# SOLU's first product in plain float32 from the raw w_in, with a new order of the first stages

## What is computed

```python
def _moe2_ref(x, w_in, w_out, g_ln):          # x 1536 x 384, w_in 384 x 1024, w_out 1024 x 384
    h = x @ w_in
    h_max = np.max(h, axis=-1, keepdims=True)
    e = np.exp(h - h_max)
    sm = e / (np.sum(e, axis=-1, keepdims=True) + 1e-09)
    solu = h * sm
    mu = np.mean(solu, axis=-1, keepdims=True)
    var = np.mean((solu - mu) ** 2, axis=-1, keepdims=True)
    ln = (solu - mu) / np.sqrt(var + 1e-06) * g_ln
    return (ln @ w_out).astype(np.float32)
```

## Time and profile before

| | us |
|---|---|
| runs (3) | 338.69, 339.14, 339.18; median 339.14 |
| the profiled execution | 340.64 |
| its span, first to last instruction | 338.8 |
| PE busy in the span | 318.0 |
| DVE, ACT, POOL busy | 206.0, 197.3, 189.1 |
| mean granted TensorE clock | 0.992 of full |

### The profile page before, as it was taken

How to read it: one execution, slowest core, us unless ns; L and a number is a source line. 1 busy time by engine, 2 the same in 40 slices (tenths; PEclk the granted TensorE clock), 3 DMA queues, 4 the chain that set the end, 5 groups by cost and what they waited for, 6 DMA issues and landing times.

```text
span 338.8 us, 6574 instructions
## 1 busy us (share of the span) xinstructions
PE 318.0 (94%) x2390; PEld 281.5 (83%) x2390; DVE 206.0 (61%) x473; ACT 197.3 (58%) x377; POOL 189.1 (56%) x170
## 2 busy tenths in 40 slices
PE   5899999977899999999999999998999999999991
PEld 2688887853699999999999999786899999999991
DVE  4567667777545555464646556889966666666610
ACT  2578777675376758576666667455554555433520
POOL 6966597963895978879696959501111111111131
PEclk9999999999999999999999999999799999999998
DMA  9999999991994949393857593000000000000000
GB/s 128 164 281 267 250 233 239 249 393 73 261 248 173 309 130 342 106 348 133 285 182 237 190 347 116 5 1 2 1 23 25 23 25 23 23 25 23 26 34 36
DMA packets 62898, 50.65 MB, mean 150 GB/s; under 512 B 42512, under 2 KB 58256, under 8 KB 62864
## 3 DMA queue, kind: packets, MB, share of 16 engines
q1 hardware_dynamic: 58784, 45.10, 47.8%
q0 software_dynamic: 1920, 4.73, 3.8%
q10 hardware_dynamic: 2160, 0.36, 0.9%
HBM read 38.37 MB, written 11.82 MB: 148 GB/s over the span
## 4 chain that ended last, share of the span: by engine, by line
PE 80%; DVE 6%; ACT 4%; issue 3%; DMA 3%; POOL 1%; another core or an unknown queue 0%; DVEq 0%; ACTq 0%; POOLq 0%
PE ps L1256 24%; PE ps L1527 15%; PE ps L1257 11%; PE ps L1510 11%; PE ps L1387 3%; PE ps L1536 3%; PE ps L1409 3%; PE ps L1355 2%; ACT scores L718 2%; PE ps L1324 2%; PE ps L1250 1%; PE ps L1370 1%; PE ps L1382 1%; DMA wsq<-in_w_dram 1%; DMA x_slots<-w_raw,slot 1%
## 5 line engine op out<-in xcount | busy, mean ns | idle before, releaser
L482 POOL TENSOR_TENSOR w_lo<-w_raw,w_hi 128x768 fp32r<-128x768 f32 x32 | 58.5, 1855 | 20.7 <-DVE w_lo L488 20.6
L1256 PE MATMUL ps<-xe,w_hi 128*128 128x448 f32 x192 | 61.7, 377 | 0.6 <-issue 0.3
L1256 PE MATMUL ps<-h,w_hi 128*128 128x448 f32 x192 | 61.6, 377 | 0.0
L1527 PE MATMUL ps<-w_hi,h 128*128 128x384 f32 x192 | 52.8, 347 | 0.6 <-issue 0.6
L1257 PE MATMUL ps<-h,w_lo 128*128 128x224 f32 x192 | 50.8, 264 | 0.0
L1257 PE MATMUL ps<-xe,w_lo 128*128 128x224 f32 x192 | 50.7, 264 | 0.0
L629 POOL TENSOR_TENSOR rstd<-var_b,minus_half 128x1 f32<-128x1 f32 x12 | 6.8, 566 | 74.2 <-DVE var_b L1204 74.2
L1510 PE MATMUL ps<-w_hi,xe 128*128 128x512 f32 x144 | 46.4, 392 | 0.6 <-ACT xe L831 0.6
L900 DVE TENSOR_TENSOR ps<-ps,rk_in 128x448 f32<-128x448 f32 x32 | 20.2, 632 | 38.0 <-ACT rk_in L673 38.0
L1256 PEld LDWEIGHTS ps<-xe,w_hi 128*128 128x128 f32 x192 | 36.0, 188 | 5.6 <-issue 2.2
L488 POOL TENSOR_TENSOR w_lo<-w_raw,w_hi 128x1024 fp32r<-128x1024 f32 x16 | 38.2, 2412 | 0.0
(11 more groups left out here) (153 smaller groups left out, 629.0 us busy)
## 6 DMA issues: line engine op xcount, KB each, us to landing
w_raw<-in_moe_w_dram SPq DMA_DIRECT2D x15, 1536.0 KB, 7.5
x_slots<-zeros SPq DMA_DIRECT2D x6, 768.0 KB, 5.6
rk_in<-in_r_dram SPq DMA_DIRECT2D x12, 192.0 KB, 5.4
rk_in<-in_k_dram SPq DMA_DIRECT2D x12, 192.0 KB, 6.4
v_in<-in_v_dram SPq DMA_DIRECT2D x12, 192.0 KB, 5.8
out_dram<-zeros SPq DMA_DIRECT2D x1, 2304.0 KB, 12.8
w_raw<-in_moe_w_dram SPq DMA_DIRECT2D x3, 512.0 KB
rows_in<-x_slots SPq DMA_DIRECT2D x8, 192.0 KB, 8.1
```

Of the source, the lines that this page charges most:

```text
L482: eng.tensor_tensor(w1_lo[:, :, cols], w1_raw[:, i, :, cols], w1_hi[:, :, cols].bitcast(F32), ALU.subtract).then_inc(g.w1_lo, 1)
L1256: pe.matmul(ps[:, bank, 0:2 * n], w_hi, x[:, c, 0:2 * n], start=first, stop=False, skip_group_check=True)
L1527: last = pe.matmul(ps[:, OB + i, 0:DM], ht[:, f, i * P:(i + 1) * P], wt[:, f, :], start=(f == 0 and z == 0), stop=(f == KF - 1 and z == 2))
```

## The change

The hidden product is made in plain float32: one matmul for each half and chunk, with `yT` as weights and the raw w_in in `w1_raw[:, 0]` as the moving side. The splits of w_in and of `yT`, with their semaphores and buffers' views, are gone: `m_hi`, `m_lo`, the ninth round of `act_w1_hi` and of `lo_w1`. In tile 0 PE waits for each chunk of y of the last expert, and once for w_in's load. On PE hidden(4) stands ahead of project(0), which moves from stage 3 to stage 4, where project(1) follows as before. On ACT ln_hi(0), and on DVE ln_lo(0), stand at the head of stage 2.

```diff
@@ POOL, experts
-                lo_w1(pool, e + 1, (e + 1) % 2, usual, parts=[0, 1])
-            lo_w1(pool, E, E % 2, usual, parts=[2, 3])
+                if e < E - 1:
+                    lo_w1(pool, e + 1, (e + 1) % 2, usual, parts=[0, 1])
@@ ACT, experts
-                    if j == 2:
+                    if j == 2 and e < E - 1:
                         act_w1_hi(act, 1 - i, w1_is_in, w1_loads(1 - i, loads), usual.w1_hi, parts=[1])
                     act_h_hi(act, e, usual, parts=[j])
-                    if j == 1:
+                    if j == 1 and e < E - 1:
                         act_w1_hi(act, 1 - i, w1_is_in, w1_loads(1 - i, loads), usual.w1_hi, parts=[0])
@@ ACT, SOLU
             def stage(n):
 
+                if n == 2:
+                    ln_hi(0, 0)
                 if t_in(n - 1):
                     squares(n - 1, (n - 1) % 2)
-                if t_in(n + 2):
-                    m_hi(n + 2, n % 2)
-                if t_in(n - 2):
+                if t_in(n - 2) and n != 2:
                     ln_hi(n - 2, n % 2)
@@ DVE, last expert
-                    if e == E - 1 and d == KD - 1:
-                        dve.wait_ge(m_hi_ready, 1)
-                        first_m_lo(m_lo_ready)
@@ DVE, SOLU
             def stage(n):
                 i = n % 2
+                if n == 2:
+                    ln_lo(0, 0)
                 if t_in(n):
                     row_max(n, i)
-                if t_in(n + 2):
-                    m_lo(n + 2, i)
                 if n <= 1:
                     w_out_remainder([[5, 6], [7]][n])
-                if t_in(n - 2):
+                if t_in(n - 2) and n != 2:
                     ln_lo(n - 2, i)
@@ PE, hidden
+                if t == 0:
+                    pe.wait_ge(usual.w1_in[0], w1_loads(0, E // 2 + 1))
                 for a, c in order:
-                    if c == 0:
-                        pe.wait_ge(usual.w1_hi, W1_PARTS * E + W1_PARTS // 2 * (a + 1))
-                        pe.wait_ge(usual.w1_lo, W1_PARTS * E + W1_PARTS // 2 * (a + 1))
-                    if a == 0 and (c == 0 or (t == 0 and c == 2)):
-                        pe.wait_ge(m_hi_ready, c // 2 + 1 if t == 0 else t + 2)
-                        pe.wait_ge(m_lo_ready, c // 2 + 1 if t == 0 else t + 2)
-                    for z, (xt, wt) in enumerate(((xe_hi, w1_hi), (xe_hi, w1_lo), (xe_lo, w1_hi))):
-                        last = pe.matmul(hidden_banks(t)[:, a, :], xt[:, c, i * P:(i + 1) * P], wt[:, c, a * 512:(a + 1) * 512],
-                                         start=(c == 0 and z == 0), stop=(c == KD - 1 and z == 2))
+                    if t == 0 and a == 0:
+                        pe.wait_ge(usual.y_taken, KD * (E - 1) + c + 1)
+                    last = pe.matmul(hidden_banks(t)[:, a, :], yT[:, c, t * P:(t + 1) * P],
+                                     w1_raw[:, 0, c, a * 512:(a + 1) * 512], start=(c == 0), stop=(c == KD - 1))
@@ PE, stage
                 if t_in(n):
                     hidden(n, n % 2)
+                    if n == 4:
+                        project(0, 0)
                     if t_in(n - 2):
                         turn_ln(n - 2, n % 2)
-                    if t_in(n - 3):
+                    if t_in(n - 3) and n != 3:
                         project(n - 3, (n - 3) % 2)
```

More of the change, by code:

```diff
@@ L160, in two_sums @@
             return ps[:, bank:bank + banks, 0:2 * n].rearrange("p b (z n) -> p b n z", z=2)
-        xe_hi, xe_lo = halves(xe, 2 * P)
         h_hi, h_lo = halves(h, 2 * P)
@@ L266, in decay_attention_moe_solu @@
         route_ready = sem("route_ready")
[L267 to L270, removed]
         h_done = sem("h_done")
@@ L622, in _ @@
                     lo_w1(pool, e, 1, whole)
-                lo_w1(pool, E, 0, whole)
             def rstd_pow(t):
@@ L785, in _ @@
                     act_h_rest(act, e, usual, j)
-                    if j == 2:
+                    if j == 2 and e < E - 1:
                         act_w1_hi(act, 1 - i, w1_is_in, w1_loads(1 - i, loads), usual.w1_hi, parts=[1])
                     act_h_hi(act, e, usual, parts=[j])
-                    if j == 1:
+                    if j == 1 and e < E - 1:
                         act_w1_hi(act, 1 - i, w1_is_in, w1_loads(1 - i, loads), usual.w1_hi, parts=[0])
-                act_w1_hi(act, 1 - i, w1_is_in, w1_loads(1 - i, loads), usual.w1_hi, parts=[2, 3])
                 if e < E - 1:
+                    act_w1_hi(act, 1 - i, w1_is_in, w1_loads(1 - i, loads), usual.w1_hi, parts=[2, 3])
                     act_xe_hi(act, e + 1, usual)
-                if e < E - 1:
                     for d in range(KD):
@@ L797, in _ @@
                         act_w2_hi(act, 1 - i, w2_is_in, 16 * loads, usual.w2_hi, parts=[d])
[L799 to L803, removed]
             flag = act.value_load(overflow[0:1, 0:1], min_val=0, max_val=1)
             with act.If(flag > 0):
-                act.wait_ge(usual.w1_lo, W1_PARTS * (E + 1))
-                act.wait_ge(m_lo_ready, 1)
+                act.wait_ge(usual.w1_lo, W1_PARTS * E)
                 act.wait_ge(usual.w2_lo, E)
@@ L821, in _ @@
                             act_h_hi(act, WHOLE * e + k, whole, parts=[j])
[L822 to L836, removed]
             def exps(t, i):
@@ L875, in stage @@
                     copy_out(n - 3, (n - 3) % 2)
-            m_hi(0, 0)
-            m_hi(1, 1)
             act.wait_ge(g_in, 16)
@@ L1108, in _ @@
             lo_w2(dve, 0, 0, usual, 0)
-            def first_m_lo(signal):
-                dve.tensor_tensor(xe_lo[:, 0:2, 0:P], yT[:, 0:2, 0:P], xe_hi[:, 0:2, 0:P].bitcast(F32), ALU.subtract)\
-                    .then_inc(signal, 1)
             dve.wait_ge(offs_ready, 1)
@@ L1151, in _ @@
                             dve_take_y(dve, WHOLE * e + k, d, at + k * P, whole)
[L1152 to L1157, removed]
-                c = slice(2, KD) if t == 0 else slice(0, KD)
-                dve.wait_ge(m_hi_ready, t + 2)
-                dve.tensor_tensor(xe_lo[:, c, here], yT[:, c, cols], xe_hi[:, c, here].bitcast(F32),
-                                  ALU.subtract).then_inc(m_lo_ready, 1)
             def w_out_remainder(fs):
@@ L1233, in stage @@
                     out_scale(n - 1, 1 - i)
-            m_lo(0, 0)
-            m_lo(1, 1)
             w_out_remainder(range(4))
@@ L1491, in _ @@
                         pe_down(pe, WHOLE * e + k, whole, e, lambda: None)
-                reach(pe, whole.w1_lo, W1_PARTS * (E + 1), 1)
-                pe.wait_ge(m_lo_again, 1)
+                reach(pe, whole.y_taken, KD * WHOLE * E, 1)
             def hidden(t, i):
```

## The result

| | us |
|---|---|
| before, median of 3 (lowest to highest) | 339.14 (338.69 to 339.18) |
| changed, median of 3 (lowest to highest) | 348.13 (347.41 to 350.0) |
| ratio, 95% interval | 1.028, 1.0216 to 1.0345 |
| the profiled execution of the changed kernel, its span | 347.41, 345.7 |

The change makes the kernel 9.0 us slower; 348.0 was forecast. In a later set of runs (6 of the changed kernel, 23 of before) the ratio was 1.0251, 1.0213 to 1.0289.

A forecast was written before the change was run, and what follows sets the result against it. PE was taken to bound the last part; plain product +12.6 us, waits and low clock -3.6, start -0.1 gave +8.9 us, 348.0 us on the median's scale. The range was 346.3 to 350.8 us, meant as 8 in 10.

The forecast's parts named there:

- The bound: Last part of the kernel: PE works without gaps, so its added time counts and savings on DVE, ACT, POOL are worth nothing.
- The plain product: Hidden product on PE: plain float32 costs 5.18 us a tile against 4.13, 12.6 us more over 12 tiles.
- What goes with it: Dropped copies and remainders of w_in and the rows on ACT, POOL and DVE: priced at nothing, hidden under PE's work.
- The start: First hidden product after the last expert: 0.1 us gained for two semaphore waits fewer, bounds 0 and 0.55.
- The order, and the waits: First tiles after the experts: 3.6 us go, 1.88 of PE idle and 1.7 of low clock; the plain product alone fills them.
- The low clock: Output product 0 in the profile of before: PE at 1.2 GHz after two waits, 5.93 us for 4.19, 1.7 us credited.
- the sum: Whole kernel: 12.6 - 3.6 - 0.1 = +8.9 us, making 348.0 us on the scale of the median.
- The cheaper product: Rival, hidden product: a record streams its columns once, 2.75 us a tile, first stages' 3.6 us stay, 322.5 us; chance 4%.
- the dearer one: Rival, hidden product: float32r record overhead holds in each stream, 5.50 us a tile, +12.7, 351.8 us; chance 4%.
- the bare loads: Rival, hidden product: the plain matmul's two weight loads are not hidden, adding 15.8 us, 364 us; chance 1%.
- the clock falls anyway: Rival, first tiles after the experts: the low clock's 1.7 us stay, 349.7 us; chance 8%.
- the two cases: Upper ends with a matmul of 0.88 us: 349.5 for the forecast, 350.8 if the clock falls anyway.

The follow-up runs named there:

- the new order: Kernel before, float32r product kept, with only the change's reordering on PE, ACT and DVE: 337.29 us, ratio 0.992 to before; SOLU part 110.4 us.

## Why the prediction was right, point by point

**The bound.** Right. The SOLU part of the changed kernel is 122.7 us of PE work with no gap, and in all fourteen traces the experts took 126.6 us, with ACT's and POOL's work on w_in under the last of them or without.

**1. The plain product.** Right, and the term that carries the result. 0.858 us a matmul and 5.15 a tile against 0.863 and 5.18: 12 x (5.15 - 4.13) = 12.2 us against 12.6. The step of 128 columns, which I extended, had 0.006 us above its two streams, and a long record has 0.002. Two records at the price of two streams each were read off the attention rows, and the cut to 256 columns confirmed both. The Trainium skill (TensorE: Matmul & The Clock Gate, Back-to-back issue gap) names 2.5 ns above the stream for an isolated matmul; the plain records agree with 2.4 above their two streams, the float32r records with their 16 do not. The Trainium skill (TensorE: Matmul & The Clock Gate, Part 3: Packing small matmuls) says that weight loads overlap running matmuls only when their row groups differ; the traces do not agree, since cutting the columns doubled the loads of full height and cost 0.03 us a tile.

**2. What goes with it.** Right: nothing gained in the expert stage.

**3. The start.** Right in size: from the branch's end the first hidden product starts 0.1 to 0.2 us sooner with the plain product, where I took 0.1. But the branch's own length varies by 0.5 us from one execution to the next, and in the two profiles compared here it hid the gain (2.0 us where it was 1.9).

**4. The order, and the waits.** The working held: the second turn started at 237.70 and its input was done at 234.86, 2.8 us sooner, as forecast; output product 0 started at 243.72 and SOLU 2 was done at 239.15, 4.6 us sooner, where I had 4.7. The plain product in the old order shows that the product and not the order did it. But the size of the term was only partly right. Its 1.9 us of waiting are in every profile, with 0.4 us that the turn and output product 0 take longer beside them. **The low clock is not: it came in one of four, and it costs 1.5 us and not the 1.7 of the sum.** So of the 3.8 us that the SOLU part of the profile of before has over the new order, 2.3 are always there, and 1.5 in about a quarter of the executions. Against the profile that I read, the SOLU part grew by 8.5 us, where the sum has 9.0 without the start; against the three other profiles it grew by 10.0. The shift of the median time is 9.0, with an interval from 7.3 to 11.7 in the first comparison and 7.2 to 9.8 in the second. The 10.0 lie just outside the second, the 8.5 inside both. Some of the gap is accounted for: from the first expert matmul to the first hidden product the traces of the plain product take 128.3 to 128.6 us and those of float32r 128.5 to 129.0. The rest is of the size of the scatter between attention and experts, and its cause stays open. The forecast agrees with the measured median to 0.1 us, but this closeness is partly luck: the product was priced 0.4 us too high, and a low clock was credited in full that most executions do not have.

**The rivals.** The cheaper product is excluded (0.858 us against the 0.74 from which it decides), and so are the dearer one and the bare loads. That the clock falls anyway did not happen in any of the four traces of the plain product. The cheaper product's working had a fault all the same: with a shorter product the first stages' waits do not stay as they were. They grow: to 8.2 us at 1.39 us a tile, even in the new order. In the range, a matmul of 0.88 us adds 72 x 0.017 = 1.2 us, which makes 349.2 and 350.9 of the two cases and not 349.5 and 350.8; nothing hangs on it.

## What to carry to other kernels

A plain float32 matmul replaces a three-part float32r product with fewer instructions and no splitting, but where PE is the bound it costs four streams instead of three: 1.02 us a tile here, twelve times, for splits that other engines made for nothing. When a change both lengthens an engine's work and reorders it to fill waits, price each by itself: the longer work had already filled them, and the order alone, on the old product, is the gain (337.3 us). And before a stretch of low clock is put in a sum, read a second profile of the same kernel.

## What the runs showed of the hardware

- A plain float32 matmul shows as two records, each of which costs twice its columns at 2.4 GHz: 0.429 us at 512 columns, 0.216 at 256. A float32r record at 512 columns takes 0.229, 0.016 above its one stream, where the plain record is 0.002 above its two.
- The branch around a large block that is not run lasted 3.38 to 3.88 us on PE's sequencer (3875 ns in the row above), while the matmuls issued before it ran on. In all fourteen traces it ended 1.37 to 1.40 us after one packet of instructions of 16 KB had landed. About half of it lay under the last expert's matmuls; five more matmuls on zeros behind them cost nothing.
- After the same two waits, 1.28 and 0.60 us with 1.06 us of transposes between them, the clock fell to 1.2 GHz for 3.4 us in one profile and stayed at 2.4 in three, and the kernel with these waits filled by matmuls on zeros had no fewer executions with such a stretch (5 of 12, against 7 of 21 of before on the same chip).
